# A fused attention and two-layer MLP kernel: the first value and weight loads are issued in another order

## The chip, the cores and the metric

The kernel runs on one core of a Trainium2 chip. The metric is the device time of one execution in microseconds (us); lower is better. A core has five instruction streams that matter here: TensorE (PE, with its weight loads PEld), VectorE (DVE), ScalarE (ACT), GpSimd (POOL) and SyncE (SP). SP computes nothing. It waits on semaphores and issues transfers, one after the other, and so its program order is the order in which the transfers are queued.

## The reference, cut to what matters

Attention over a band of 96 keys and a few global ones, for 2 batches of 8 heads, 768 positions and 64 channels, and behind it two MLPs over the 1536 rows:

```python
scores = scale * q @ k.T + bias          # bias: per-head slope times distance
keep   = is_global | is_local            # local: 0 <= i - j < 96, global: j < 8
a = softmax(where(keep, scores, -1e9))
x = (a @ v) reshaped to [1536, 512]
h = x @ w_in1;  x = (h * sigmoid(h)) @ w_out1          # d_ff = 2048
h = x @ w_in2;  y = (h * clip(h + 3, 0, 6) / 6) @ w_out2
```

## The kernel before

**Attention.** Two heads share the 128 partitions, so there are NPAIR = 8 head pairs (`it` counts them), each with NT = 6 tiles of 128 queries. A tile is a unit `u`, of which there are 48. PE takes them two at a time: `scores(r)` (line 1076) computes the scores of units 2r and 2r + 1. The steady loop `for m in range(2, NM)` in PE's `banded` then does, for each m: `scores(2m)`, `scores(2m + 1)`, the transposes of the probabilities (`turn_pair`, line 1100), the products with v (`values(2m - 4)` and `values(2m - 3)`, line 1124) and the transposes of the inverse sums (`turn_inverses`, line 1109). DVE adds the bias and takes the row maximum, ACT takes the exponential and copies transposes out of PSUM, POOL sums and, between, prepares the first MLP weights (`W_WORK`: what POOL does with them behind which `r`).

**Which transfer feeds what.** Every pair has three loads: k (`load_k`, 464 KB), q (`load_q`, 384 KB) and v (`load_v`, 704 KB), each in one of two buffers by `it % 2`. `scores(r)` waits for k and q where a pair begins, which is at r = 3 (pair 1), r = 6 (pair 2), r = 9 (pair 3) and so on. `values(r)` waits for v at the same r. `scores(6)` is the first thing that PE does in the round m = 3, `scores(9)` stands in the round m = 4.

**MLP.** 32 steps s = 0 to 31 of 256 hidden columns. A step uses one block of w_in (`load_wi(s)`, 512 KB into `wi_raw[:, s % 2]`) and one of w_out (`load_wo(s)`, 512 KB). `load_wi(s)` first waits until block s - 2 has been split into its high and low part; for s = 0 and 1 neither load waits. POOL begins on block 0 of w_in behind r = 4, on block 1 behind r = 9, and ACT begins on block 0 of w_out in the round m = 5.

**SP's program.** It issues the small counts, pair 0's k in two pieces, waits for the first of these and issues k of pair 1. Meanwhile ACT's queue issues q of pair 0 in two pieces and q of pair 1. Then SP waits for a flag from DVE (whether the counts fit the banded program) in `either`, branches to `banded` and goes on as below. `s_done` counts finished `scores(r)`, `pv_done` finished `values(r)`; HALF is 3.

```python
sp.wait_ge(k_in[1], NQK)                 # k of pair 1 has landed
load_v(sp, 0)
load_wi(sp, 0)
for it in range(2, NPAIR):
    sp.wait_ge(s_done, HALF * (it - 1))
    load_qk(sp, it)
    if it > 2:
        sp.wait_ge(pv_done, HALF * (it - 2))
    load_v(sp, it - 1)
    if it == 3:
        load_wi(sp, 1); load_wo(sp, 0); load_wo(sp, 1)
```

In these terms the order is: v0, w_in block 0, k2, q2, v1, then k3, q3, v2, w_in block 1, w_out blocks 0 and 1, and so on.

Of the kernel before, what the change touches and what calls it, by code (L numbers as in the profile page):

```python
# [64 lines left out]
def at_least(eng, sem, value):  # L65

    if isinstance(value, int) and value <= 0:
        return
    eng.wait_ge(sem, value)


def build(nc, qT, kT, v, w_in1, w_out1, w_in2, w_out2, counts, out):
    outer = ExitStack()
    with outer:
# [124 lines left out]
        def load_k(eng, it):  # L199
            eng.dma_start(k_raw[it % 2][:, 0:KW], kT[it]).then_inc(k_in[it % 2], 16)  # L200
# [4 lines left out]
        def load_qk(sp, it):  # L205
            load_k(sp, it)
            load_q(sp, it)
# [4 lines left out]
        def load_v(sp, it):  # L212
            sp.dma_start(v_raw[it % 2][:, :, :, :], v[it]).then_inc(v_in[it % 2], 16)

        def load_wi(sp, s):
            at_least(sp, wi_lo_ok, 2 * (s - 1))
            w = w_in1 if s < NSTEP // 2 else w_in2
            sp.dma_start(wi_raw[:, s % 2, 0:4 * QC], w[s % STEPS]).then_inc(wi_in[s % 2], 16)

        def load_wo(sp, s):  # L220
            at_least(sp, wo_lo_ok, s - 1)
            w = w_out1 if s < NSTEP // 2 else w_out2
            sp.dma_start(wo_raw[:, s % 2, :], w[s % STEPS]).then_inc(wo_in[s % 2], 16)
# [5 lines left out]
        def either(eng, banded, general):  # L229

            eng.wait_ge(flag_ok, 1)
            fits = eng.value_load(flag[0:1, 0:1], min_val=0, max_val=1)  # L232
            with eng.If(fits):
                banded()
            with eng.Else():
                general()
# [3 lines left out]
        @block.sync  # L240
        def _(sp):
            sp.dma_start(words[:, :], counts).then_inc(words_in, 16)
            sp.dma_start(k_raw[0][:, 0:K_FIRST], kT[0][:, 0:K_FIRST]).then_inc(k_first, 16)
            sp.dma_start(k_raw[0][:, K_FIRST:KW], kT[0][:, K_FIRST:KW]).then_inc(k_in[0], 16)

            sp.wait_ge(k_first, 16)
            load_k(sp, 1)

            def first_w():
                for s in range(2):  # L250
                    load_wi(sp, s)
                    load_wo(sp, s)

            def banded():

                sp.wait_ge(k_in[1], NQK)
                load_v(sp, 0)
                load_wi(sp, 0)

                for it in range(2, NPAIR):  # L260
                    sp.wait_ge(s_done, HALF * (it - 1))
                    load_qk(sp, it)
                    if it > 2:
                        sp.wait_ge(pv_done, HALF * (it - 2))
                    load_v(sp, it - 1)
                    if it == 3:
                        load_wi(sp, 1)
                        load_wo(sp, 0)
                        load_wo(sp, 1)
                sp.wait_ge(pv_done, HALF * (NPAIR - 2))  # L270
                load_v(sp, NPAIR - 1)

            def general():
                load_v(sp, 0)
                with sp.Fori(1, NPAIR) as it:
                    sp.wait_ge(a_pv, 2 * NT * it)
                    sp.dma_start(k_raw0[:, 0:KW], kT[it]).then_inc(k_in[0], 16)
                    sp.dma_start(q_raw0[:, :], qT[it]).then_inc(q_in[0], 16)
                    sp.dma_start(v_raw0[:, :, :, :], v[it]).then_inc(v_in[0], 16)
                first_w()  # L280
            either(sp, banded, general)

            def store(b, t):
                sp.wait_ge(y_dve if t % 2 else y_act, HALF * (2 + b) + t // 2 + 1)
                sp.dma_start(out[b, t], y_out[:, t, :]).then_inc(stored, 16)
            load_wi(sp, 2)
            for s in range(2, NSTEP):
                if s + 1 < NSTEP:
                    load_wi(sp, s + 1)
                load_wo(sp, s)  # L290
                if s == 3 * STEPS + 3:
                    for t in range(NT):
                        store(0, t)
            for i, t, cols in LAST:
                dve_before = sum(j < i for j in LAST_DVE)
                if i in LAST_DVE:
                    sp.wait_ge(y_dve, HALF * 3 + dve_before + 1)
                else:
                    sp.wait_ge(y_act, HALF * 3 + i - dve_before + 1)
                sp.dma_start(out[1, t][:, cols], y_out[:, t, cols]).then_inc(stored, 16)  # L300
            sp.wait_ge(stored, 16 * (NT + len(LAST)))
# [1032 lines left out]
```

## Time and profile before

| | before |
|---|---|
| median of 3 runs | 586.84 us (586.80 to 586.97) |
| the profiled execution's own time | 586.97 us |
| its span, first to last instruction | 585.2 us |
| PE busy | 580.0 us, 99% of the span |
| DVE / ACT / POOL busy | 361.9 / 335.5 / 266.7 us |
| moved by DMA | 50.05 MB, mean 86 GB/s |

The page of the profile gives the busy time of each engine, and behind it the chain of work that ended last: at each step back, the instruction or the transfer that released the one in question. An engine that is busy nearly all the time and makes up nearly all of that chain is the bound. Attention takes about the first 87 us, the MLPs the rest. The other views used are the waits (which engine stood idle until which other one had finished), the timeline (instructions in order of time, runs of equal ones merged), the transfers (issue to landing) and busy time by stretch.

### The profile page before, as it was taken

What the parts mean: (1) busy time and instruction counts of PE and PEld (TensorE: products, weight loads), DVE (VectorE), ACT (ScalarE), POOL (GpSimd) and SP (SyncE); (2) the same over time, 40 slices, a digit from 0 to 9 for tenths busy, and PEclk for the clock granted to TensorE, in tenths of its full rate; (3) what the DMA queues carried; (4) which work ended last, traced back from release to release, by engine and by line L of the source; (5) the groups of instructions that cost most, each with busy time, mean ns of one, the idle gap of its engine ahead of it and who ended that gap; (6) DMA issues with size and microseconds to landing.
All of it is one profiled execution on the core that took longest, in us unless ns stands there. A gap on an engine that the chain in (4) does not pass through costs nothing.

```text
span 585.2 us, 9670 instructions
## 1 busy us (share of the span) xinstructions
PE 580.0 (99%) x3476; PEld 522.5 (89%) x3476; DVE 361.9 (62%) x669; ACT 335.5 (57%) x652; POOL 266.7 (46%) x282
## 2 busy tenths in 40 slices
PE   9999999999999999999999999999999999999998
PEld 6788899999999999999999989999988988889996
DVE  7777887657545775586556685475448765555331
ACT  7998976554444774444447575445546754455441
POOL 6678774678333044394333343593330443331110
DMA  6665500422222122212221222222211262211002
GB/s 238 256 237 191 204 7 2 144 72 73 73 73 72 36 73 73 73 43 101 73 72 37 73 72 73 74 72 73 71 46 30 70 216 72 71 37 38 1 0 108
DMA packets 14883, 50.05 MB, mean 86 GB/s; under 512 B 1650, under 2 KB 2162, under 8 KB 14834
## 3 DMA queue, kind: packets, MB, share of 16 engines
q1 hardware_dynamic: 14402, 48.63, 24.5%
q10 hardware_dynamic: 432, 0.79, 0.4%
q8 instruction: 28, 0.46, 0.3%
q14 instruction: 21, 0.17, 0.1%
HBM read 46.27 MB, written 3.15 MB: 84 GB/s over the span
## 4 chain that ended last, share of the span: by engine, by line
PE 97%; DVE 1%; ACT 1%; issue 0%; DMA 0%; DVEq 0%
PE ps L1152 40%; PE ps L1243 23%; PE ps L1234 15%; PE ps L1235 8%; PE ps L1100 3%; PE ps L1124 3%; PE ps L1076 3%; PE ps L1109 1%; ACT probs L842 1%; DVE negs L623 0%; DMA words<-in_counts 0%; ACT probsT L853 0%; DVEq L232 0%; DVE m_base L568 0%; DVE x_raw L641 0%
## 5 line engine op out<-in xcount | busy, mean ns | idle before, releaser
L404 POOL TENSOR_TENSOR wo_lo<-wo_raw,wo_hi 128x1024 fp32r<-128x1024 f32 x32 | 77.3, 2415 | 260.1 <-ACT wo_hi L907 257.0
L1152 PE MATMUL ps<-x_hi,wi_hi 128*128 128x384 f32 x448 | 150.8, 337 | 0.1
L1152 PE MATMUL ps<-x_hi,wi_lo 128*128 128x384 f32 x448 | 150.0, 335 | 0.0
L1152 PE MATMUL ps<-x_lo,wi_hi 128*128 128x384 f32 x448 | 150.0, 335 | 0.0
L599 DVE TENSOR_TENSOR c_sb<-ps,p_c 128x384 f32<-128x384 f32 x64 | 35.6, 557 | 161.7 <-PE ps L1152 161.5
L887 ACT ACTIVATE p_c<-ps 128x384 f32<-128x384 f32 x64 | 31.5, 492 | 127.4 <-PE ps L1152 127.1
L1152 PEld LDWEIGHTS ps<-x_hi,wi_hi 128*128 128x128 f32 x448 | 84.1, 188 | 3.4 <-ACT u_c L887 0.9
L1152 PEld LDWEIGHTS ps<-x_hi,wi_lo 128*128 128x128 f32 x448 | 84.1, 188 | 0.7
L1152 PEld LDWEIGHTS ps<-x_lo,wi_hi 128*128 128x128 f32 x448 | 84.1, 188 | 0.0
L1243 PE MATMUL ps<-wo_hi,g_lo 128*128 128x512 f32 (+1 forms) x194 | 76.3, 393 | 0.0
L1243 PE MATMUL ps<-wo_lo,g_hi 128*128 128x512 f32 (+1 forms) x194 | 76.3, 393 | 0.0
L1243 PE MATMUL ps<-wo_hi,g_hi 128*128 128x512 f32 (+1 forms) x194 | 76.2, 393 | 0.0
L996 ACT ACTIVATE g_hi<-g_f 128x768 fp32r<-128x768 f32 x64 | 50.6, 838 | 42.3 <-DVE g_f L609 24.8
L581 DVE TENSOR_TENSOR wi_lo<-wi_raw,wi_hi 128x896 fp32r<-128x896 f32 x60 | 66.8, 1152 | 0.0
L865 ACT ACTIVATE wi_hi<-wi_raw 128x896 fp32r<-128x896 f32 x60 | 53.6, 937 | 0.0
L1234 PE MATMUL ps<-g_hi,wo_hi 128*128 128x512 f32 x128 | 50.0, 391 | 0.0
L1234 PE MATMUL ps<-g_lo,wo_hi 128*128 128x512 f32 x128 | 50.0, 391 | 0.0
L1234 PE MATMUL ps<-g_hi,wo_lo 128*128 128x512 f32 x128 | 50.0, 390 | 0.0
L842 ACT ACTIVATE probs<-negs,negmax 128x256 f32<-128x256 f32 (+1 forms) x96 | 45.8, 481 | 3.8 <-DVE negmax L623 3.7
L1243 PEld LDWEIGHTS ps<-wo_hi,g_lo 128*128 128x128 f32 x194 | 36.4, 188 | 8.6
L1243 PEld LDWEIGHTS ps<-wo_hi,g_hi 128*128 128x128 f32 x194 | 36.4, 188 | 8.0
L1243 PEld LDWEIGHTS ps<-wo_lo,g_hi 128*128 128x128 f32 x194 | 36.5, 188 | 8.0
(113 smaller groups left out, 1064.3 us busy)
## 6 DMA issues: line engine op xcount, KB each, us to landing
wi_raw<-in_w_in SPq DMA_DIRECT2D x32, 512.0 KB, 3.4
wo_raw<-in_w_out SPq DMA_DIRECT2D x32, 512.0 KB, 3.4
v_raw<-in_v SPq DMA_DIRECT2D x8, 704.0 KB, 4.0
k_raw<-in_kT SPq DMA_DIRECT2D x7, 464.0 KB, 5.1
out_y<-y_out SPq DMA_DIRECT2D x11, 256.0 KB, 4.1
q_raw<-in_qT SPq DMA_DIRECT2D x6, 384.0 KB, 6.0
q_raw<-in_qT ACTq DMA_DIRECT2D x1, 384.0 KB, 4.6
k_raw<-in_kT SPq DMA_DIRECT2D x1, 320.0 KB, 3.7
```

The source lines that it names most:

```text
L404: nc.gpsimd.tensor_tensor(wo_lo[:, s % 2, :], wo_raw[:, s % 2, :], wo_hi[:, s % 2, :], ALU.subtract).then_inc(wo_lo_ok, 1)
L581: nc.vector.tensor_tensor(wi_lo[:, s % 2, at], wi_raw[:, s % 2, QC + 7 * P * part:QC + 7 * P * part + 7 * P], wi_hi[:, s % 2, at], ALU.sub ...
L599: nc.vector.tensor_tensor(c_sb[:, i, :], p_bank(bank), add[:, :], ALU.add).then_inc(c_ok, 1)
L842: nc.scalar.activation(probs[:, u % DEEP, h, a:256], negs[:, u % 3, h, a:256], ACT.Exp, bias=negmax[:, u % DEEP, h:h + 1], scale=-1.0, acc ...
L865: nc.scalar.activation(wi_hi[:, s % 2, at], wi_raw[:, s % 2, QC + 7 * P * part:QC + 7 * P * part + 7 * P], ACT.Copy).then_inc(wi_hi_ok, 1)
L887: nc.scalar.activation(dst[:, :], p_bank(bank), ACT.Copy).then_inc(kept, 1)
L996: nc.scalar.activation(g_hi[:, s % 2, f, :], g_f[:, f, :, :].rearrange("p a t -> p (a t)"), ACT.Copy, scale=1.0 if s < NSTEP // 2 else 1.0 ...
L1076: mm = nc.tensor.matmul(s_bank(u, h)[:, 0:width], q_raw[it % 2][D * h:D * h + D, P * t:P * t + P], k_raw[it % 2][D * h:D * h + D, first:fi ...
L1152: mm = nc.tensor.matmul(p_bank(bank), w[:, s % 2, at], x[:, b, k, :], start=fresh and k == 0 and i == 0, stop=k == 1 and i == 2, skip_grou ...
L1234: nc.tensor.matmul(y_bank(i), wo[:, s % 2, w], g[:, s % 2, c, 0:512], start=first, stop=last)
L1235: mm = nc.tensor.matmul(y_bank(4 + i // 2)[:, 256 * (i % 2):256 * (i % 2) + 256], wo[:, s % 2, w], g[:, s % 2, c, 512:S], start=first and ...
L1243: mm = nc.tensor.matmul(y_bank(t)[:, cols], g[:, s % 2, c, P * t:P * t + P], wo[:, s % 2, DM * c + cols.start:DM * c + cols.stop], start=s ...
```

## The change

v of pair 0 is issued behind k of pair 1, before SP waits for the flag and for the landing of that k. Behind the landing SP issues v of pair 1 (which had stood behind k and q of pair 2), and then all four first weight blocks, of which three had stood at `it == 3`. k and q of pair 2 come behind them. The number of transfers and their sizes are the same. No other engine's program is touched.

```diff
             sp.wait_ge(k_first, 16)
             load_k(sp, 1)
+            load_v(sp, 0)
...
             def banded():
-
                 sp.wait_ge(k_in[1], NQK)
-                load_v(sp, 0)
-                load_wi(sp, 0)
+                load_v(sp, 1)
+                first_w()
 
                 for it in range(2, NPAIR):
                     sp.wait_ge(s_done, HALF * (it - 1))
                     load_qk(sp, it)
                     if it > 2:
                         sp.wait_ge(pv_done, HALF * (it - 2))
-                    load_v(sp, it - 1)
-                    if it == 3:
-                        load_wi(sp, 1)
-                        load_wo(sp, 0)
-                        load_wo(sp, 1)
+                        load_v(sp, it - 1)
...
             def general():
-                load_v(sp, 0)
                 with sp.Fori(1, NPAIR) as it:
```

`first_w` is `for s in range(2): load_wi(sp, s); load_wo(sp, s)`. The function `general` is the program for other counts and doesn't run on these inputs.

On SP, from the load of k of pair 1 (the first row) to the loads of k and q of pair 3, the program before reads as follows; 128x928 is k, 128x768 is q, 128x1408 is v, and each row is one transfer:

```order
L200 DMA k_raw<-in_kT 128x928 [waits k_first]
L232 TENSOR_LOAD flag [waits flag_ok]
L232 ISA x2
L233 COMPARE_AND_BRANCH
L213 DMA v_raw<-in_v 128x1408 [waits k_in1]
L218 DMA wi_raw<-in_w_in 128x1024
L200 DMA k_raw<-in_kT 128x928 [waits s_done]
L203 DMA q_raw<-in_qT 128x768
L213 DMA v_raw<-in_v 128x1408
L200 DMA k_raw<-in_kT 128x928 [waits s_done]
L203 DMA q_raw<-in_qT 128x768
```

And with the change, the same stretch of SP's program, which now ends one pair earlier, at the loads of k and q of pair 2:

```order
L200 DMA k_raw<-in_kT 128x928 [waits k_first]
L213 DMA v_raw<-in_v 128x1408
L232 TENSOR_LOAD flag [waits flag_ok]
L232 ISA x2
L233 COMPARE_AND_BRANCH
L213 DMA v_raw<-in_v 128x1408 [waits k_in1]
L218 DMA wi_raw<-in_w_in 128x1024
L223 DMA wo_raw<-in_w_out 128x1024
L218 DMA wi_raw<-in_w_in 128x1024
L223 DMA wo_raw<-in_w_out 128x1024
L200 DMA k_raw<-in_kT 128x928 [waits s_done]
L203 DMA q_raw<-in_qT 128x768
```

Between the wait for k of pair 1 and q of pair 2 there were two other transfers, v0 and one weight block; now there are five, v1 and four weight blocks.

## Rows read from the trace of the kernel before

**Rows 1.** The page: busy time of PE, and the chain by engine.

```profile
PE 580.0 (99%) x3476; PEld 522.5 (89%) x3476; DVE 361.9 (62%) x669; ACT 335.5 (57%) x652; POOL 266.7 (46%) x282
...
PE 97%; DVE 1%; ACT 1%; issue 0%; DMA 0%; DVEq 0%
```

**Rows 2.** Waits of PE, 0 to 110 us: total us, times, longest.

```profile
PE ps L1058 <- DVE y_out L517: 1.1, 1, 1.1
PE ps L1109 <- DVE x_raw L641: 0.4, 1, 0.4
PE ps L1124 <- issue: 0.3, 1, 0.3
PE ps L1100 <- ACT probs L842: 0.2, 1, 0.2
```

**Rows 3.** Timeline of PE: start, duration in us, instructions, idle before.

```profile
9.55 0.93 PE L1076 MATMUL ps<-k_raw,q_raw 64*128 64x128 f32 x8
...
16.01 1.75 PE L1124 MATMUL ps<-probsT,v_raw 128*64 128x128 f32 x28 [0.34 <-issue]
...
19.49 1.79 PE L1076 MATMUL ps<-k_raw,q_raw 64*128 64x128 f32 x16
```

**Rows 4.** Timeline of SP, its transfers: start us, us.

```profile
3.89 0.33 SPq L200 DMA_DIRECT2D k_raw<-in_kT  x1
8.73 0.33 SPq L213 DMA_DIRECT2D v_raw<-in_v  x1
...
10.06 0.68 SPq L203 DMA_DIRECT2D q_raw<-in_qT  x1
10.79 0.46 SPq L213 DMA_DIRECT2D v_raw<-in_v  x1
...
14.62 0.43 SPq L203 DMA_DIRECT2D q_raw<-in_qT  x1
23.37 0.33 SPq L213 DMA_DIRECT2D v_raw<-in_v  x1
...
29.98 0.33 SPq L213 DMA_DIRECT2D v_raw<-in_v  x1
```

**Rows 5.** Transfers issued at 3.89, 8.73, 10.06, 10.79, 14.62, 29.98: KB, us to landing.

```profile
k_raw<-in_kT SPq DMA_DIRECT2D x1, 464.0 KB, 4.8
...
v_raw<-in_v SPq DMA_DIRECT2D x1, 704.0 KB, 4.4
...
q_raw<-in_qT SPq DMA_DIRECT2D x1, 384.0 KB, 6.5
...
v_raw<-in_v SPq DMA_DIRECT2D x1, 704.0 KB, 7.5
...
q_raw<-in_qT SPq DMA_DIRECT2D x1, 384.0 KB, 6.4
...
v_raw<-in_v SPq DMA_DIRECT2D x1, 704.0 KB, 6.4
```

**Rows 6.** Busy us by stretch (engines in order, PEclk, DMA share, GB/s).

```profile
7.00:9.00 2.00, 2.00 (x15) 0.98 (x13) 1.96 (x11) 1.94 (x9) 1.24 (x4) 1.00 0.07 26
20.00:24.00 4.00, 4.00 (x49) 3.25 (x48) 3.34 (x19) 3.95 (x17) 3.63 (x8) 1.00 0.01 4
25.00:31.00 6.00, 6.00 (x69) 5.01 (x68) 4.70 (x22) 5.22 (x20) 4.36 (x7) 1.00 1.00 377
```

**Rows 7.** The chain that ended last, 18 to 33 us: start, us, what.

```profile
19.56 1.72 PE ps L1076 x16
...
25.52 1.72 PE ps L1076 x16
...
31.45 1.71 PE ps L1076 x13
```

**Rows 8.** Line 1076 from 4 to 8 us, then 19 to 22: ns min/median/max.

```profile
L1076 PE MATMUL ps<-k_raw,q_raw x10: 461/631/631, 5.8 to 7.9; 64*128 64x256 f32 x10
...
L1076 PE MATMUL ps<-k_raw,q_raw x16: 272/376/378, 19.5 to 20.9; 64*128 64x256 f32 x12, 64*128 64x128 f32 x4
```

## The prediction, made before the changed kernel ran

> **What bounds the kernel now.** I read the page first: PE is busy 580.0 of 585.2 us and makes up 97% of the chain that ended last [rows 1]. Nothing else matters unless it makes PE wait, or ends a wait of PE. So the second view is PE's waits over the first 110 us, which hold attention, the only part in which the moved transfers land. They sum to 2.0 us, and none ends on a transfer: two end on DVE, one on ACT, one on nothing that the profile shows [rows 2]. The 1.1 us at the start is the kernel's first instruction. There is no wait for data that an earlier transfer could take away. The third step is to ask of each moved transfer when it lands and when PE wants it; the timeline of PE and of SP and the landing times answer that [rows 3 to 5].
>
> **v0, issued earlier.** It was issued at 8.73 and landed 4.4 us later, at 13.1 [rows 4, 5]. Its reader is the first product with v, at 16.01 [rows 3]. It was 2.9 us early already, so landing sooner gives nothing. It does fill a hole: from 7 to 9 us the DMA engines are busy 7% of the time [rows 6], because SP sits waiting for k1. Behind k1, v0 (704 KB, at the rate found below some 1.8 us) fits into that hole and is through by about 9.0. The instruction costs SP one issue of 0.33 us while it has nothing else to do but wait: nothing on the path.
>
> **v1, issued earlier.** It takes v0's place: 704 KB issued at 8.73 as soon as k1 has landed. In the trace before, it landed at 10.79 + 7.5 = 18.3 [rows 4, 5]; its first use is values(3), in the round that begins at 19.56 [rows 7], so nothing is gained here either.
>
> **The weight blocks.** Three of 512 KB go from the transfers behind 23.37 [rows 4] to those behind 8.73. PE waits for no transfer in that later stretch, so their leaving it ends no wait. A busy DMA system might still have slowed PE by contention. The chain answers that: the round that begins at 19.56 takes 5.96 us with DMA idle for most of it, the next one 5.93 us with DMA busy all the time at 377 GB/s [rows 6, 7]. The same round with and without traffic differs by 0.03 us. Value of clearing the later stretch: zero; a gain of more than a few times 0.03 us is excluded.
>
> **k2 and q2, which come later.** This is the term that counts. scores(6) opens the round m = 3 and needs k2 and q2. Before, q2 landed at 10.06 + 6.5 = 16.6 and PE took up scores(6) at 19.49 [rows 3 to 5], so there were 2.9 us of slack. Now q2 stands behind v1, w_in 0, w_out 0, w_in 1, w_out 1 and k2. Counted from the issue at 8.73, that is 704 + 4 x 512 + 464 + 384 = 3600 KB up to and with q2, where it was 704 + 512 + 464 + 384 = 2064 KB.
>
> When does the 3600th KB of such a burst land? Three readings of the same trace:
> 1. The first burst itself. Up to and with q3 it moves v0, w_in 0, k2, q2, v1, k3, q3 = 3616 KB without a gap, and q3 landed at 14.62 + 6.4 = 21.0, which is 12.3 us behind the issue at 8.73 [rows 4, 5]. For 3600 KB: 21.0.
> 2. The second burst, which has three weight blocks in it, as the new one has four. From v2's issue at 23.37 to v3's landing at 29.98 + 6.4 = 36.4 it took 13.0 us for v2, three blocks, k4, q4 and v3 = 3792 KB. Less 192 KB (0.5 us) that is 12.5 us, or 21.2.
> 3. The fastest run of it: from v0's landing (13.1) to q2's (16.6) came 1360 KB in 3.4 us, 396 KB a us. At that rate all the way, 13.1 + 2896/396 = 20.4.
>
> I take 21.1, between the first two, since they are whole bursts of the same length. Ends: 20.4 and, below, 22.2. With 0.04 us for the wake-up (SP issued v0 at 8.73, k1 had landed at 8.69) PE starts scores(6) at 21.1 where it could have started at 19.49: **a stall of 1.6 us**, 0.9 at the low end.
>
> How much of it reaches the end? PE executes in order, and all that stands behind scores(6) waits too. From the chain's rows the rounds that follow are wholly PE's [rows 7], and in 20 to 24 us PE is busy 4.00 of 4.00 [rows 6]. There is no idle time in which it could catch up; I count 0 to 0.2 us regained. POOL, ACT and DVE have less to do than PE and cannot hurry it. So 1.6 us go through.
>
> **k3, q3 and v2.** k3 and q3 are issued on scores(5)'s completion, q3 at 14.62 as before, and land behind q2, 848 KB or 2.3 us later, at 23.4. scores(9) is the second item of the next round, which began at 25.5 before [rows 7] and begins at 27.1 now. Covered by 3 us and more. v2 and what follows find an emptier queue than before. The two weights for POOL and ACT are wanted long after: block 0 of w_in now lands behind v1, exactly where it landed behind v0, and the others earlier than before.
>
> **k1, with something behind it.** scores(3) needs it at 9.55 [rows 3]; it landed at 3.89 + 4.8 = 8.69 [rows 4, 5]. Before, nothing stood behind it, now v0 does. In the first burst transfers landed one after another with later ones behind them, in the order of issue, so the likely cost is zero. If instead the engines shared themselves evenly between k1 and v0, k1's 464 KB would take as much of v0 along: 464/396 = 1.2 us. PE would start scores(3) at 9.9 instead of 9.55 (0.35 us), SP would issue the burst 1.2 us later, q2 would land at about 22.3 against a need moved to 19.84, and the sum would be 0.35 + 2.4 = 2.8 us. That is my upper end without a change of clock.
>
> **The sum.** Profiled execution 586.97 + 1.6 = 588.6; the three runs' median is 586.84, 0.13 lower, so 588.4 for the median, 0.27% above.
>
> **Rivals.**
> A, **the cover holds**: q2 lands in time or almost, and nothing is measured. The place is scores(6) alone; it decides at a landing by 19.5, and shows as no change up to a stall of 1.2 us, that is a landing by 20.7. For it: the 20.4 of the third reading, and v0 now runs before the burst, so that v1 may start without the slow first microsecond. Against: both whole bursts say 21.0 and more. Time: 586.8 to 587.9, at the rate of the third reading 587.8.
> B, **faster**: the hole from 7 to 9 us is filled and the later burst is thinner. It would need 1.2 us of PE waits on transfers, or of contention; rows 2 have none of the first, rows 7 show 0.03 us of the second. Time if all of the 0.9 us of PE's idle between 1.2 us and 110 us went: 585.9.
> C, **k1 is delayed as well**: 2.8 us, 589.6, by the even sharing above.
> D, **the stall costs the clock**. The granted clock stands at 1.00, the 2.4 GHz level, in every stretch that I read [rows 6]. Yet the first score matmuls, up to 7.9 us, took 631 ns where the later ones of the same shape take 376 [rows 8], 1.68 times as long: the engine came from standing still. If PE fell back to that pace after the stall and took as long to recover as at the start, about 7 us of wall time would hold 7/1.68 = 4.2 us of work: 2.8 us more, 588.4 + 2.8 = 591.2. Against: its gaps of 0.2 to 0.4 us [rows 2, 3] were followed by full pace. No gap as long as 1.6 us is in this stretch, so the rows don't exclude it.
> The Trainium skill, "TensorE: Matmul & The Clock Gate", Part 1, says that a throttled clock is the default and that activity releases it, between 1.2 and 2.4 GHz. By that rule the slow start is the rest state; the durations of the first matmuls agree (631 against 376 ns), the clock column doesn't show it, and D is what the rule would do here if the stall counted as rest.
>
> **How the numbers follow.** My forecast, 1.6 us of stall passed through (any sum of 1.2 to 2.2), 0.55. A 0.26. B 0.04. C 0.10. D 0.05. A difference under about 0.2%, 1.2 us, can't be told from none here. Slower by more: 0.55 + 0.10 + 0.05 = 0.70; within: 0.26; faster: 0.04. The range leaves out D, B and the outermost of A and C: 587.0 to 589.8. The likeliest case is 588.4.
>
> **What the profile would show.** Right: PE's waits gain one row in which line 1076 stands idle for a transfer, k or q, 1.5 us long, at 19.5 us; q2 lands at 21.1; every later round has its length of 5.9 to 6.1 us and starts 1.6 us later; the end moves by as much. v0 landed by 10.5, v1 at 13.1, and POOL doesn't wait for w_in. Wrong: no such row (A); scores(3) later than 9.55 (C); score matmuls of 631 ns behind 21 us (D); a later round that is shorter, so that the stall is won back. The weakest step is the landing of q2: 0.5 us less and the result can't be told from none.

## The result and the profile after

The changed kernel takes 590.04 us (median of 7 runs, 588.30 to 593.34), the kernel before 586.86 us (median of 7, 586.80 to 587.10). The ratio is 1.0061, with a 95% interval of 1.0036 to 1.0087: slower by 3.2 us. The direction was forecast, the size was not: twice the 1.6 us, and outside the range of 587.0 to 589.8. Something else is new in these numbers. The runs before lie within 0.3 us, the runs after within 5 us. The profiled execution took 590.93 us, its span is 589.2 us, 4.0 more than before.

PE's waits over the whole execution, the counterpart of [rows 2] (engine, line, what it waited for: total us, times, longest; line 1076 is now 1071, since the file is five lines shorter):

```profile
PE ps L1071 <- DMA q_raw<-in_qT: 2.5, 1, 2.5
PE ps L1053 <- DVE y_out L512: 1.1, 1, 1.1
PE ps L1071 <- DVE negmax L618: 0.5, 1, 0.5
```

There is the forecast row: line 1071 stands idle for q, once, but for 2.5 us and not 1.5. The timeline of PE shows where, as [rows 3] did (start, duration, instructions, idle before):

```profile
18.81 0.63 PE L1104 MATMUL ps<-ident,rinv 128*128 128x128 f32 x4 [0.36 <-DVE x_raw L636]
21.95 2.40 PE L1071 MATMUL ps<-k_raw,q_raw 64*128 64x128 f32 x16 [2.51 <-DMA q_raw<-in_qT]
24.29 1.97 PE L1095 MATMUL ps<-ident,probs 128*128 128x128 f32 x8
26.18 1.83 PE L1119 MATMUL ps<-probsT,v_raw 128*64 128x128 f32 x28
27.95 1.09 PE L1095 MATMUL ps<-ident,probs 128*128 128x128 f32 x8
28.91 0.63 PE L1104 MATMUL ps<-ident,rinv 128*128 128x128 f32 x4
29.46 1.79 PE L1071 MATMUL ps<-k_raw,q_raw 64*128 64x256 f32 x16
```

scores(6) starts at 21.95 where it had started at 19.49. Look at the durations behind it. The same 16 score matmuls take 2.40 us and not 1.79, the first eight transposes 1.97, while the next eight take 1.09. The round from scores(6) to scores(8) lasts 29.46 - 21.95 = 7.51 us; before it lasted 5.95. Busy time by stretch says why, in the column behind the five engines, the granted clock (the last two are DMA share and GB/s; compare [rows 6], where it is 1.00):

```profile
20.00:22.00 2.00, 0.05 (x2) 0.08 (x2) 0.00 (x0) 0.95 (x3) 1.76 (x5) 1.00 1.04 401
22.00:24.00 2.00, 2.00 (x16) 1.62 (x16) 0.99 (x7) 0.57 (x3) 0.79 (x1) 0.75 0.40 143
24.00:26.00 2.00, 2.00 (x10) 1.57 (x8) 1.83 (x12) 0.87 (x4) 0.78 (x2) 0.50 0.00 0
26.00:28.00 2.00, 2.00 (x31) 1.65 (x29) 0.69 (x1) 1.99 (x9) 0.83 (x2) 0.90 0.00 0
```

PE stood still until 21.95; from about 23 to 26.4 us it was granted half its clock, 1.2 GHz. So the loss has two parts: 2.51 us of stall and 7.51 - 5.95 = 1.56 us of slow clock. Less the 0.05 us by which PE reached the place earlier, that is 4.02 us, the whole of the 4.0 us between the spans. Nothing further is lost or won behind 29.5 us.

One more row is new, the 0.5 us of line 1071 behind DVE. It stands in front of scores(3), which starts at 9.88 and not at 9.55:

```profile
9.88 0.93 PE L1071 MATMUL ps<-k_raw,q_raw 64*128 64x128 f32 x8 [0.50 <-DVE negmax L618]
```

That is the sign that rival C named. The profile puts the wait down to DVE, but k1 landed in the same tenth of a microsecond, at 9.79, so which of the two held PE is not decided. It cost nothing at the end: PE was at scores(6) 0.05 us earlier than before.

The chain that ended last now passes through the transfers (start, us, what), where that of before was PE's alone [rows 7]:

```profile
3.59 6.20 DMA k_raw<-in_kT
...
9.80 0.33 SPq L213
...
12.83 8.98 DMA q_raw<-in_qT
21.82 0.14 issue
21.95 2.40 PE ps L1071 x16
```

k1 landed 6.2 us after its issue (4.8 before, [rows 5]), at 9.80 and not at 8.69; SP started the burst there, and q2, behind it, landed at 21.82.

### The profile page after: what moved, and what is told of

Read it like the earlier page. It is cut to its first block, busy times and chain, and to the rows that moved or that the text cites. A ratio compares the mean times of both kernels' runs of the same rounds, so it can differ in the third digit from the quotient of the medians.

```text
span 589.2 us, 9670 instructions
## 1 busy us (share of the span) xinstructions
PE 580.8 (99%) x3476; PEld 523.2 (89%) x3476; DVE 361.7 (61%) x669; ACT 335.5 (57%) x652; POOL 267.1 (45%) x282
## 4 chain that ended last, share of the span: by engine, by line
PE 96%; DMA 3%; SPq 1%; issue 0%; DVE 0%
PE ps L1147 40%; PE ps L1238 23%; PE ps L1229 15%; PE ps L1230 8%; PE ps L1095 3%; PE ps L1119 3%; PE ps L1071 3%; DMA q_raw<-in_qT 2%; DMA k_raw<-in_kT 1%; PE ps L1104 1%; SPq L218 0%; SPq L223 0%; SPq L200 0%; DVE y_out L818 0%; SPq L242 0%
```

## The experiments

All times are medians; a granted clock is the mean over an execution, and 0.997 is what the fall above leaves of 1.000. The kernel before ran at 586.8 us beside every group; one of its runs took 588.12.

**Is it the place of k2 and q2?** One edit in the changed kernel, which puts k2 and q2 in front of three of the four weight blocks:

```diff
                 load_v(sp, 1)
-                first_w()
+                load_wi(sp, 0)
                 for it in range(2, NPAIR):
                     sp.wait_ge(s_done, HALF * (it - 1))
                     load_qk(sp, it)
+                    if it == 2:
+                        load_wo(sp, 0)
+                        load_wi(sp, 1)
+                        load_wo(sp, 1)
```

> The changed kernel with one thing put back: k2 and q2 stand in front of three of the four weight blocks (order: v0 early, v1, w_in 0, k2, q2, w_out 0, w_in 1, w_out 1). All else of the change stays, and the same bytes have moved by the end of the burst. Theory 1 (only the place of k2 and q2 matters): q2 has 2064 KB up to and with it, lands at 16 to 17.6, no wait of PE for a transfer, granted clock 1.00; 586.7 to 587.1, as before, every run. Theory 2 (four weight blocks and their traffic early cost time by themselves, by contention or through k3 and q3): over 588.

Measured: 586.82 us over 10 runs (586.76 to 587.24), ratio 1.0000 (0.9991 to 1.0010). PE waits for no transfer, and scores(6) starts at 19.37. v0 early, v1 early and all four weight blocks early, with the same traffic, cost nothing, and they gain nothing. All of the loss hangs on what stands in front of k2 and q2.

**v0 alone.** The kernel before, with `load_v(sp, 0)` moved behind `load_k(sp, 1)` and nothing else:

> The kernel before, with only v0 moved: it is issued behind k1, before the flag. Question: does v0 behind k1 delay k1, and does that cost time by itself? In the changed kernel k1 landed 6.2 us after its issue instead of 4.8. Theory 1 (v0 shares the DMA engines with k1): k1 lands at about 9.8 again, scores(3) starts 0.3 us late at 9.9, but PE has caught up by scores(6) at 19.4 to 19.5; q2 has only w_in 0 and k2 before it, lands near 16.5 and is early; time as before, 586.6 to 587.2. Theory 2 (the delay of k1 is passed on to the end, as my rival C said): 587.2 or more. If k1 lands at 8.7 here, its delay in the changed kernel came from something else.

Measured: 586.82 us over 10 runs, ratio 1.0001 (0.9992 to 1.0010), scores(3) at 9.31, no wait for a transfer. k1 landed after 4.2 us, so theory 1 was wrong on that: v0 behind it did not delay it here. v0 is off the path, as forecast.

**The weights alone.** The kernel before, with the three other weight blocks moved in front of k2 and q2, v0 and v1 where they were:

```diff
                 load_v(sp, 0)
-                load_wi(sp, 0)
+                first_w()
...
-                    if it == 3:
-                        load_wi(sp, 1)
-                        load_wo(sp, 0)
-                        load_wo(sp, 1)
```

> The kernel before, with only the three other weight blocks moved in front of k2 and q2; v0 stays behind the wait for k1, v1 behind q2. 3600 KB up to and with q2, as in the change, but the burst starts at 8.73 and not at 9.80. Theory 1 (the transfers in front of q2 are the cause, and the stall starts the clock's fall): q2 lands at 20.8 to 21.0, a stall of 1.3 to 1.6 us at scores(6); if the granted clock then falls as in the changed kernel, 1.5 us more, so 589.7 to 590.1 and runs that scatter over 2 us and more; in executions without a fall 588.2 to 588.5. Theory 2 (the stall is handed on once and the clock stays): 588.2 to 588.5 in all runs. Theory 3 (the cause is k1's delay by v0): 587.

Measured: 588.75 us over 6 runs, 587.73 to 591.11, ratio 1.0041 (1.0027 to 1.0056). The highest run has a clock of 0.997. The profiled run is the lowest:

```profile
20.31 1.79 PE L1072 MATMUL ps<-k_raw,q_raw 64*128 64x128 f32 x16 [0.57 <-DMA q_raw<-in_qT]
```

v0 was issued at 8.27 and q2 landed at 11.46 + 8.7 = 20.2, 11.9 us behind it. The 12.3 us that I had read from the first burst before were about right; the stall is short because k1 landed earlier, and because PE came to the place 0.25 us later. The weights alone make 2.0 of the 3.2 us and a scatter of 3.4 us. The clock has little part in it: only one of the six runs fell. Runs of 588.33, 589.18 and 589.61 us, 1.5 to 2.8 us above before, have a clock of 1.000.

**704 KB less and 704 KB more in front of q2.** The changed kernel with v1 behind q2 again, and the changed kernel with v0 at the head of the burst:

> The changed kernel with v1 behind q2 again: 2896 KB up to and with q2, 704 KB less than in the change. In the trace of the change 3600 KB took 12.0 us from the first issue to q2's landing; by 704/390 it is 1.8 us less, 10.2. The landing of k1, from which the burst starts, was between 7.9 and 9.8 in the traces so far. Theory 1 (the stall is what is left over of the landing of q2 behind 19.4): q2 lands between 18.1 and 20.0; a stall of 0 to 0.6 us; 586.8 to 587.4. If the clock's fall needs a stall of some length, hardly a run shows it. Theory 2 (a fall can follow any stall): some runs at 588.5 and more.

Measured: 587.01 us over 11 runs (586.83 to 588.43), ratio 1.0008 (0.9999 to 1.0017). In the profiled run q2 landed at 10.90 + 8.2 = 19.1, PE did not wait. Seven of the runs lie within 0.3 us of before, four at 587.3 to 588.4: the landing falls close to the edge. All eleven have a clock of 1.000.

> The changed kernel with v0 not issued early but as the first of the burst: 4304 KB up to and with q2, 704 more than in the change. Theory 1 (stall = landing of q2 less 19.4, then the clock): q2 lands 1.8 us later than in the change, at 21.8 to 23.6; a stall of 2.4 to 4.1 us; without a fall of the clock 589.2 to 591, and with one (1.5 to 3.4 us) up to 594; median about 592.5, about 2.5 us above the change. The early v0 is then worth 1.8 us by keeping 704 KB out of the burst. Theory 2 (the early v0 harms by delaying k1): this kernel is as fast as the change or faster.

Measured: 591.81 us over 4 runs, 589.26 to 593.07, ratio 1.0091 (1.0076 to 1.0107); three of the four have a clock of 0.994 to 0.997. The profiled run (clock 1.00) has a stall of 2.39 us. q2 landed at 11.85 + 9.8 = 21.7, no later than the 21.8 in the changed kernel. So the 1.8 us that an early v0 was to save don't show in the landing. I come back to it below.

**A stall without a transfer.** The kernel before with its transfers as they were; PE only waits, in front of scores(6), for a copy that ACT ends later:

```diff
                 for m in range(2, NM):
+                    if m == 3:
+                        pe.wait_ge(inverses_ok, 2)
                     scores(2 * m)
```

> The kernel before with its transfers untouched; PE only waits in front of scores(6) until ACT has copied the second set of inverse sums, which ended at 21.07 in the trace before. A stall of about 1.6 us at the same place with no transfer in it. Theory 1 (any stall of this length costs its own length, and then the clock): stall 1.6 us, granted clock under 1.00 behind it in some executions or all, time 588.4 (no fall) to 590.1 (fall), with scatter. Theory 2 (the slow matmuls behind the stall come from the DMA traffic): clock 1.000, time 588.4 within 0.3 us.

> e5_wait_without_dma once more, to have more executions beside e8_wait_with_pe_busy, which had one group of runs (588.5 to 588.7) where e5 had two (three at 588.4, two at 590.1 to 590.3). Theory 1 (a stall of 1.56 us brings a fall of the clock in some executions): again two groups, a third to a half of the runs at 590.1 to 590.3 and a clock of 0.996 to 0.997. Theory 2 (the two high runs were chance): all at 588.4.

Measured: 588.49 and 588.48 us. The ten runs fall into two groups: six at 588.40 to 588.49 with a clock of 1.000, four at 590.13 to 590.28 with 0.996 to 0.997. Each set's profile caught one group. First the one without a fall, then one with it:

```profile
21.01 1.79 PE L1076 MATMUL ps<-k_raw,q_raw 64*128 64x128 f32 x16 [1.56 <-ACT inverses L858]
```

```profile
21.16 3.36 PE L1076 MATMUL ps<-k_raw,q_raw 64*128 64x128 f32 x16 [1.56 <-ACT inverses L858]
```

The same stall of 1.56 us, and behind it the same 16 matmuls in 1.79 or in 3.36 us. Busy time by stretch of the second one:

```profile
20.00:22.00 2.00, 0.84 (x6) 0.84 (x8) 0.00 (x0) 1.10 (x5) 1.76 (x5) 0.75 0.00 0
22.00:24.00 2.00, 2.00 (x12) 1.45 (x10) 1.05 (x7) 0.63 (x3) 0.93 (x1) 0.50 0.00 0
24.00:26.00 2.00, 2.00 (x22) 1.39 (x20) 1.74 (x13) 1.11 (x4) 0.77 (x2) 0.89 0.00 0
```

The DMA engines are idle here (the last two columns), so the slow matmuls don't come from traffic. The stall passes through whole: 588.4 - 586.8 = 1.6 us. The two profiled spans differ by 1.75 us. Of this, 1.56 us is the slow round: scores(8) starts 28.66 - 21.16 = 7.50 us behind scores(6), in the other profile 26.95 - 21.01 = 5.94. Another 0.15 us was there before scores(6) began.

**The same stall with PE at work.** As above, but PE fills the wait with four matmuls into a PSUM region that scores(6) then overwrites (the profile counts each of them twice, as x8):

```diff
                     if m == 3:
+                        pe.wait_ge(neg_done, 4 * (2 * m - 1))
+                        for _ in range(4):
+                            nc.tensor.matmul(s_bank(12, 0), y_out[:, 0, 0:P],
+                                             v_raw[0][:, 0, 0:4, :], start=True, stop=True)
                         pe.wait_ge(inverses_ok, 2)
```

> The same wait without a transfer as in e5_wait_without_dma (PE waits for ACT's copy of the second inverse sums, 1.56 us), but PE fills it with 4 matmuls of 128x256 (about 1.2 us of work) into a PSUM region that scores(6) overwrites, and then waits for the rest. e5 gave two groups of runs, 588.4 at a granted clock of 1.00 and 590.1 to 590.3 at 0.996. Theory 1 (the fall comes from PE standing still): all runs 588.4 to 588.6, clock 1.00. Theory 2 (the fall comes from the shift in time, not from the idleness): again two groups. The extra matmuls of e4_pe_kept_busy ended only at 22.76 and brought a gap of 2.1 us in the MLP part, so that run doesn't answer this.

Measured: seven runs, all between 588.51 and 588.73. The upper group is gone.

```profile
19.24 1.89 PE L1174 MATMUL ps<-v_raw,y_out 128*128 128x256 f32 x8
21.07 1.79 PE L1076 MATMUL ps<-k_raw,q_raw 64*128 64x128 f32 x16
```

scores(6) starts as late as in the stall (21.07 against 21.01 and 21.16), after matmuls and not after idleness. With a fall in 4 of 10 executions as above, seven in a row without one have a chance of 0.6^7 = 3%. But the 4 of 10 are a small sample too, taken in other groups of runs: if both kernels fell equally often, 4 falls among these 17 executions would all be in the first ten in 9% of cases.

**A shorter stall.** The wait is `pe.wait_ge(exp_done, 24)` in place of the wait for the inverse sums:

> The kernel before with a shorter wait of PE without a transfer: in front of scores(6) it waits until ACT has done the exponentials of unit 11, which ended at 20.5 in the trace before: 1.0 us instead of 1.56. Theory 1 (a stall passes through whole, and the fall of the clock needs a longer one): all runs 587.8 to 587.9, clock 1.00. Theory 2 (any stall may bring a fall): some runs at 589.5.

Measured: stall 1.08 us in the profiled run, eleven runs at 587.89 to 588.18, none raised, ratio 1.0018 (1.0009 to 1.0027). The stall passes through whole (587.98 - 586.80 = 1.18) and brings no fall.

**The changed kernel with PE at work, and once more as it is.** First attempt, 15 matmuls of 128x128:

> The changed kernel, in which PE has 15 extra 128x128 matmuls in front of scores(6), into a PSUM region that scores(6) then overwrites; they fill the wait for q2. Extra work on PE, 15 x 0.165 = 2.5 us, all in the time in which it stood still (2.5 us). Theory 1 (the clock falls because PE stands still, and that is 1.5 us and more of the loss, and all of the scatter): granted clock 1.00 throughout, scores(6) still at about 21.95, the runs agree within 0.5 us, time 588.9 to 589.4, so 0.6 to 1.5 us faster than the changed kernel in spite of more work. Theory 2 (the clock's fall has nothing to do with the standing still): clock 0.997 as before, 590 to 591 with scatter.

Measured: 592.90 us (590.24 to 593.82), ratio 1.0101 (1.0083 to 1.0118), and a clock of 0.997 in three of six runs. It does not decide between the theories. The matmuls took 3.51 us, not 2.5, and ended behind q2's landing. The profiled run also has a gap of PE in the MLP that no other kernel here has:

```profile
PE ps L1147 <- issue: 2.1, 1, 2.1
```

Its page also has one more instruction fetch (29 on queue 8, 28 before). PE has 30 matmuls more; that the gap is a late fetch was not tested, nor whether the three lower clocks stand behind that gap. The times would fit it. PE took up scores(6) at 22.76, 3.4 us later than the 19.4 of most other traces, which makes 590.2, and the fastest run took 590.24. With the gap of 2.1 us that is 592.3, and two runs with a clock of 1.000 took 592.13 and 592.21. The three with the lower clock took 593.58 to 593.82, which is room for the gap and a fall of about 1.4 us, while a fall without the gap would be near 591.7. The second attempt has the four larger matmuls from above:

> The changed kernel with 4 matmuls of 128x256 (1.9 us in e8_wait_with_pe_busy) in front of scores(6), which fill the wait for q2; e4_pe_kept_busy had 15 smaller ones, which took 3.5 us and ran past the landing. Theory 1 (standing still brings the fall): PE takes up scores(6) at 21.1 to 22, all runs between 588.5 and 589.5, none at a granted clock under 0.999; the changed kernel's runs up to 593 are gone. Theory 2 (the fall has another cause): runs of 590 and more with a clock of 0.997 and less remain, as many as in a2_change_again.

> The changed kernel once more, beside the experiments. In its first trace k1 landed 6.2 us after its issue, in all traces of the experiments 4.1 to 4.5, and the burst in front of q2 starts with k1's landing. Theory 1 (the late k1 is a matter of the execution, the burst takes its 12 us in any case): where k1 lands at about 8.1, q2 lands at 20.0 to 20.4, the stall is 0.6 to 1.0 us and the run 587.7 to 588.1 at a granted clock of 1.00; where k1 or the burst are later, the stall is up to 2.5 us, and some of the longer stalls bring a fall of the clock, 590 and more. Median 587.9 to 590. Theory 2 (v1 and v0 together make k1 late in every execution of this kernel): k1 again lands at 9.8, the stall is 2.5 us.

Measured: the changed kernel again 591.69 us over 6 runs, 588.26 to 593.12, ratio 1.0068 (1.0043 to 1.0092), four of the six with a clock of 0.994 to 0.997. With PE at work 589.43 us over 5 runs, 588.82 to 589.86, ratio 1.0042 (1.0029 to 1.0055), all with a clock of 1.000. With four matmuls that nobody needs the median is 2.3 us lower than without them in the same group of runs, and 1.2 us lower than that of all 14 executions of the changed kernel (590.6). The intervals of the two ratios overlap, so that gain is not certain. The missing falls are clearer: none in 5 here, against 9 in the 14 of the changed kernel. If PE's work made no difference, chance would put all 9 among the 14 in 2% of cases, and this and the result of the stall without a transfer together would come up in 0.2%. The profiled run of the changed kernel again:

```profile
22.01 3.36 PE L1071 MATMUL ps<-k_raw,q_raw 64*128 64x128 f32 x16 [2.49 <-DMA q_raw<-in_qT]
25.30 1.97 PE L1095 MATMUL ps<-ident,probs 128*128 128x128 f32 x8
...
30.61 1.79 PE L1071 MATMUL ps<-k_raw,q_raw 64*128 64x256 f32 x16
```

Its stall is as long as in the first trace, but the granted clock was at 1.2 GHz for twice as long, from about 20.9 to 27.7 us (0.72, 0.50, 0.50 and 0.58 over the four stretches of 2 us from 20 on), where it had been 3.4 us: the round takes 30.61 - 22.01 = 8.60 us, 2.65 more than the 5.95 before. 2.49 + 2.65 is 5.1 of the 5.2 us between its span of 590.4 and 585.2. Its chain shows when k1 and q2 landed, at 8.71 and 21.88:

```profile
3.76 4.95 DMA k_raw<-in_kT
...
12.44 9.44 DMA q_raw<-in_qT
21.88 0.14 issue
```

With PE at work, the same place reads:

```profile
19.27 1.89 PE L1169 MATMUL ps<-v_raw,y_out 128*128 128x256 f32 x8
22.02 1.79 PE L1071 MATMUL ps<-k_raw,q_raw 64*128 64x128 f32 x16 [0.86 <-DMA q_raw<-in_qT]
```

scores(6) starts at the same time, 22.0, and at full speed.

## Why the prediction was right and wrong

**Right: the place and the mechanism.** No wait for v0, v1 or the weights was there to take away; the only thing on the path was the landing of q2 against scores(6). Moving k2 and q2 forward gives 586.82 us, and moving 704 KB out of their way 587.01.

**Right: the stall passes through whole.** 1.08 us of idleness cost 1.18 us, 1.56 us cost 1.6 us. The rounds that follow have their length of 5.9 to 6.1 us, and none wins anything back. With all transfers as before and the wait on ACT instead, the cost is the same, so it is the idleness that is paid for and not the traffic.

**Right: contention is nothing.** The fourth term, clearing the later stretch, was put at zero. The kernel with k2 and q2 first clears it too and measures the same as before.

**Wrong: the size of the stall.** I had 1.6 us from a landing at 21.1. The five executions of the changed kernel whose clock stayed at 0.999 or more took 588.26 to 589.50 us, which is a stall of 1.4 to 2.7 us; both profiles show 2.5. In the four profiles with this order of transfers (the change twice, and with four and with 15 matmuls) q2 landed at 21.8, 21.9, 21.9 and 21.6. Another 0.14 us from the landing to the first matmul, the "issue" of the chain, was not in my sum. The burst's length was well read for the first trace (12.0 us from the first issue to q2's landing, 12.3 forecast). The start was not: k1 landed at 9.80. That is rival C's place, and it has a part of the first trace: 1.07 us. In the second trace k1 landed after 4.9 us, at 8.7, and the burst took 13.1 us. The step that failed is "v0 is through by about 9.0": I let it vanish into the hole in front of the burst at no cost to what stands behind. Its last part landed at 11.5 and 10.4 us in the two traces of the change, behind the 9.8 and 8.7 at which the burst began.

The trace's landing records of the 16 parts of each transfer show more. In the second trace of the change the middle part of q2 (the eighth of 16 in order of landing) landed 1.1 us earlier than in the kernel with v0 in the burst. Counted from the landing of k1 it is 1.6 us, near the 1.8 that the bytes would have. But the last part was 2.1 us behind the middle one, where it was 0.8 us there, and PE waits for the last. From v1 to q2, the last part of every transfer came 2.1 to 2.2 us behind its middle one, and 1.4 to 1.9 us behind all the others. That it is each time the same DMA engine is likely, but the records don't name the engine. The same reading over the profiles: with v0 early the last part of q2 was 0.8 to 2.5 us behind the middle one (1.3 and more in six of seven), with v0 in its old place 0.6 to 0.9 in seven of seven. So the early v0 saves the bytes and gives them back in this lag; in these two profiles that is why the landing in the kernel with v0 in the burst is no later. The Trainium skill, "DMA: Bandwidth & Descriptors", "Queues, rings and completion order", says that a transfer is split over up to 16 rings, one on each DMA engine, and that transfers need not complete in the order in which they were issued. The records agree with the split, in parts that land up to 2.5 us apart; the transfers in front of q2 did land in order. Why one part falls behind was not tested. Nor is the landing of k1 settled: 4.8 us after its issue before, 4.1 to 4.5 in the experiments, four with v0 behind it among them, and 4.9, 5.5 and 6.2 in the change, twice, and in the change with four matmuls.

**Wrong: the clock.** Rival D had a chance of 0.05 and happened in 9 of 14 executions of the changed kernel. This is the step that carried the result out of the range: with 2.1 us of stall and no fall the median would be 588.9. Its price was of the right size but rather high: I had 2.8 us from the slow pace of the first matmuls [rows 8]; measured are 1.56 and 2.65 us in the two profiles, and 1.56 us again in the stall without a transfer. What failed is the evidence that I set against it: gaps of 0.2 to 0.4 us followed by full pace say nothing of one of 1.6 us. I wrote that the rows don't exclude it, and then weighed it as if they nearly did. Idleness of 1.08 us: a fall in 0 of 11 executions. Of 1.56 us: 4 of 10. Of 1.4 to 2.7 us with the burst: 9 of 14. Of 2.4 us and more with v0 in the burst: 3 of 4. Against this stand the weights alone, 1 of 6, with three unfallen runs 1.5 to 2.8 us above before, and v1 back, 0 of 11, with two runs 1.5 and 1.6 us above. The first four counts rise with the length of the stall, the last two show that the length alone does not decide it. What does is not shown.

Together: median 590.04 = 586.8 + about 2 us of stall (the middle of the five executions without a fall is 2.1) + the fall in somewhat more than half of the executions. In hindsight, with D at half instead of a twentieth, the same working gives 588.4 or 590 to 591 with about equal weight, and a range that holds the result.

**What stays open.** Why k1 lands anywhere from 4.1 to 6.2 us after its issue; why the last part of a transfer lags; what decides between a fall and none in executions of the same kernel; and what the 2.1 us gap of PE in the kernel with 15 matmuls is.

No version here beats the kernel before. The order with k2 and q2 first equals it.

## What to carry to other kernels

In a queue that is served in order, a transfer's price is paid by what stands behind it: list, for each transfer moved forward, the ones that it passes and how early those were. Count the bytes in front of each from the same starting point, and read the time for that many bytes from a burst of the trace; then add a margin, since the start and the last of the engines scatter by 1 to 2 us. In a kernel like this one, bound by TensorE, a stall costs its own length, and one of 1.5 us and more may cost as much again in clock. If it can't be avoided, a few matmuls in it that nobody needs may be cheaper than the idleness. Here no execution with them fell, in 12, and in the changed kernel the median was 1.2 us lower, though so few runs don't make that gain sure; 15 of them, which ran past the end of the wait, made it worse.

## What the runs showed of the hardware

- A single idle stretch of TensorE of 1.56 us, in a stage in which it is busy otherwise, brought the clock from 2.4 to 1.2 GHz in 4 of 10 executions of the same kernel. The slow stretch cost 1.56 us in two profiles, with the clock down for 3.4 us, and 2.65 us in a third, with the clock down for 6.8 us, of which PE stood still for 1.1. Beside the scatter of q2's landing, it is why the changed kernel spreads over 5 us where the one before spread over 0.3.
- The Trainium skill, "TensorE: Matmul & The Clock Gate", "HAM oscillation — how this bites in real kernels", describes a thin kernel whose waits for DMA throttle the engine again and again. Here a single wait for a transfer did it, and a wait for ACT did it as well.
- The fall may come behind the stall and not in it: in the first trace PE resumed at 21.95 at full clock, and the clock fell at about 23; in the other two profiles with a fall it was down when PE resumed.
- The time from issue to landing of a transfer is that of its slowest part. In a burst of 3600 KB the last of 16 parts came to land 2.1 us behind the middle one. For q2 this lag was 1.3 us and more only where v0 was issued early, in six profiles of seven.
